# Ranking of the cluster marks one step later, for heads 3 to 15, in a fused clustered-attention and two-layer MLP kernel

## The reference

```python
q_assign = np.argmax(np.einsum('bhsd,hcd->bhsc', q_n, c_n), axis=-1)
k_assign = np.argmax(np.einsum('bhsd,hcd->bhsc', k_n, c_n), axis=-1)
mask = q_assign[:, :, :, None] == k_assign[:, :, None, :]
scores = scale * np.matmul(q, k.transpose(0, 1, 3, 2))
scores = np.where(mask, scores, -1000000000.0)
...
attn = attn / (np.sum(attn, axis=-1, keepdims=True) + 1e-09)
return np.matmul(attn, v)
# then (P(h) / Q(h)) @ w_out with h = x @ w_in, P a cubic and Q = 1 + |b0||h| + |b1|h^2
# then (silu(x @ w_gate) * (x @ w_val)) @ w_out
```

## Time and profile before

| What | Value |
|---|---|
| median of 3 runs | 780.21 us (780.07 to 780.3) |
| the profiled execution, its own time | 779.8 us |
| its span, first to last instruction | 778.0 us |
| busy: PE, DVE, ACT, POOL | 773.2, 569.0, 516.3, 523.1 us |
| DVE busy, attention stretch (slices 1 to 10 of 40) | 90% and more in most slices |
| granted TensorE clock | full in all 40 slices |
| scores of tile 95, the last | at 228.00 us of the span |

### The profile page before, as it was taken

One profiled execution on the slowest core, in us unless ns is written; L12 is line 12 of the kernel. 1 busy time (PEld: TensorE's weight loads), 2 busy tenths in 40 slices (PEclk: granted clock), 3 DMA queues, 4 the chain that ended last, 5 costly groups with the idle time before them and its releaser, 6 DMA issues.

```text
span 778.0 us, 12682 instructions
## 1 busy us (share of the span) xinstructions
PE 773.2 (99%) x4231; PEld 700.5 (90%) x4231; DVE 569.0 (73%) x1046; ACT 516.3 (66%) x960; POOL 523.1 (67%) x457
## 2 busy tenths in 40 slices
PE   9999999999999999999999999999999999999998
PEld 8999999999998888888888888899999999999997
DVE  6999999999998787777777777644544555554554
ACT  7888888888888787686777789553554444333322
POOL 4878999998575997222222488879888975665610
PEclk9999999999999999999999999999999999999999
DMA  8857665463402600000000111341212214211002
GB/s 189 196 138 183 166 175 139 118 163 90 121 14 82 190 0 1 1 0 1 1 0 1 29 44 38 95 122 55 55 28 55 55 29 134 55 42 41 27 1 82
DMA packets 57521, 57.53 MB, mean 74 GB/s; under 512 B 6576, under 2 KB 44272, under 8 KB 57456
## 3 DMA queue, kind: packets, MB, share of 16 engines
q1 hardware_dynamic: 57296, 56.32, 26.9%
q10 hardware_dynamic: 160, 0.39, 0.2%
HBM read 33.59 MB, written 3.15 MB: 47 GB/s over the span
## 4 chain that ended last, share of the span: by engine, by line
PE 98%; DVE 1%; issue 0%; ACT 0%; POOL 0%; POOLq 0%
PE ps L1310 19%; PE ps L1311 19%; PE ps L1312 19%; PE ps L1464 8%; PE ps L1481 4%; PE ps L1408 4%; PE ps L1409 4%; PE ps L1483 4%; PE ps L1407 4%; PE ps L1445 4%; PE ps L1450 4%; PE ps L1515 2%; PE ps L1306 1%; DVE neg_max L1191 1%; DVE probT_lo L1217 0%; PE ps L1419 0%
## 5 line engine op out<-in xcount | busy, mean ns | idle before, releaser
L599 POOL TENSOR_TENSOR den<-den,mag 128x512 f32<-128x512 f32 x48 | 62.4, 1300 | 120.1 <-ACT den L780 119.9
L1312 PE MATMUL ps<-x_hi,w_lo 128*128 128x512 f32 (+1 forms) x384 | 139.5, 363 | 0.0
L658 POOL TENSOR_TENSOR w_lo<-w_raw,w_hi 128x768 fp32r<-128x768 f32 (+1 forms) x48 | 101.6, 2125 | 56.3 <-ACT w_hi L839 56.3
L1310 PE MATMUL ps<-x_hi,w_hi 128*128 128x512 f32 (+1 forms) x384 | 139.4, 363 | 0.0
L1311 PE MATMUL ps<-x_lo,w_hi 128*128 128x512 f32 (+1 forms) x384 | 139.4, 363 | 0.0
L680 POOL TENSOR_SCALAR prob<-prob,row_inv 128x768 f32<-128x768 f32 x96 | 85.9, 912 | 28.0 <-DVE row_inv L1207 27.1
L1217 DVE TENSOR_TENSOR probT_lo<-ps,probT_hi 128x384 fp32r<-128x384 f32 x192 | 97.3, 548 | 6.1 <-ACT probT_hi L927 5.1
L927 ACT ACTIVATE probT_hi<-ps 128x384 fp32r<-128x384 f32 x192 | 83.7, 489 | 22.7 <-PE ps L1464 21.4
L1191 DVE TENSOR_REDUCE neg_max<-ps 128x1 f32<-128x768 f32 x96 | 90.9, 948 | 1.1 <-PE ps L1450 0.8
L907 ACT ACTIVATE prob<-ps,neg_max 128x768 f32<-128x768 f32 x96 | 86.7, 904 | 2.9 <-DVE neg_max L1191 2.7
L1464 PE MATMUL ps<-ident,prob 128*128 128x128 f32 x576 | 79.8, 274 | 0.2
(11 more groups left out here) (150 smaller groups left out, 1988.8 us busy)
## 6 DMA issues: line engine op xcount, KB each, us to landing
w_raw<-in_moe_w_gate SPq DMA_DIRECT2D x48, 128.0 KB, 2.3
w_raw<-in_moe_w_val SPq DMA_DIRECT2D x48, 128.0 KB, 2.6
k_hihi<-qk_hi SPq DMA_DIRECT2D x31, 192.0 KB, 3.3
w_raw<-in_moe_w_in SPq DMA_DIRECT2D x16, 256.0 KB, 3.5
w_raw<-in_moe_w_out SPq DMA_DIRECT2D x16, 256.0 KB, 4.5
qk_raw<-in_q SPq DMA_DIRECT2D x16, 192.0 KB, 4.0
qk_low<-qk_hi SPq DMA_DIRECT2D x16, 192.0 KB, 3.7
qk_low<-qk_lo SPq DMA_DIRECT2D x16, 192.0 KB, 4.1
```

Source lines behind the costliest of these rows:

```text
L658: did(g.tensor_tensor(lo[:, wave, :], raw[:, wave, :], hi[:, wave, :].bitcast(F32), ALU.subtract), s_w2lo)
L1310: mm(dst, hi, m_hi, start=start, stop=False)
L1312: return mm(dst, lo, m_hi, start=False, stop=stop)
```

## The change

In heads 3 to 15 VectorE takes the marks behind the sum of x of step 4, instead of ahead of that step's maximum. Their transposes move from the end of step 4 to the end of step 5, the copy from the start of step 5 to the start of step 0, the rank from step 5 to the end of the transposes of step 0, and the two `cluster` instructions from the end of step 5 to the end of step 0. No instruction is added or removed. SyncE's and GpSimd's orders are the same; SyncE's six DMAs for the rows wait for the later `cluster`.

```diff
-    STAGES = (0, 2, 8, 8, 8, 8, 10, 10, 11, 11)
+    STAGES = (0, 2, 8, 8, 8, 8, 10, 11, 12, 12)
...
                 h = early_at(step, S_CLUSTER)
                 if h is not None:
                     cluster(h)
-                h = steady_at(step, S_MARKS)
-                if h is not None:
-                    marks(h)
                 maximum(step)
...
                 if not products_first(step):
                     x_sum(step)
+                h = steady_at(step, S_MARKS)
+                if h is not None:
+                    marks(h)
                 h = steady_at(step, S_CLUSTER)
                 if h is not None:
                     cluster(h)
...
                 if products_first(step):
                     products(step)
                     turn(step)
-                else:
-                    turn(step)
                     h = steady_at(step, S_RANK)
                     if h is not None:
                         order(h)
+                else:
+                    turn(step)
                     products(step)
```

## The result

The changed kernel takes **781.78 us**, the median of 15 runs (781.49 to 781.96). The kernel before took 780.07 us in 15 runs beside it (779.94 to 780.44). The ratio is 1.0021, with a 95% interval of 1.0014 to 1.0028: the change makes the kernel 1.7 us slower. The forecast was 782.5, with slower as the likeliest outcome.

The account below looks back on a forecast made before the run. TensorE's queue plus its waits was taken as the bound. Terms 1.40 + 0.84 = 2.24, about 2.3, gave 778.0 + 2.3 = 780.3 of span, 782.1 with 1.8 around it, and 0.4 for the median: 782.5 us, range 780.0 to 784.4.

Parts of the forecast that it names:

- Term (c): Cluster instructions behind step 0's low parts: VectorE late through steps 1 to 3, TensorE waits 0.12 in seven heads, 0.84 us.
- term (a): Between step 4's last product and step 5's first: 1.44 us of work left to cover a 1.65 chain, 1.40 us lost.
- The reading of the bound: TensorE's instruction queue plus its waits sets the time; adding and removing no instruction, the change can only move waits.
- The tail's pattern: Steps 88 to 89 and 95, without a rank: transposes to product 0.79 (upper partitions) and 0.72 (lower), waits 0.21 and 0.14.
- The hold of VectorE's sum: Late start of the sum of x, 1.04 against 0.92 behind the low parts, expected to travel with the sum.
- Term (b): Marks' transposes and rank in their new places, steps 5 and 0: same work, marks and copy in time, cost 0.
- Term (d): Six row DMAs on SyncE starting later, still landed before the scores that read them: cost 0.
- Rival 1: Only the lost cover before step 5's product costs; VectorE's slack absorbs the later cluster instructions: 781.6 us, chance 0.23.
- Rival 2: Sum of x, no longer behind the marks, ends in time; seven heads' 0.13 wait goes: 779.3 us, chance 0.10.
- Rivals 3: VectorE as the bound: its 0.4 can't be made up; logits or steps 2 to 4 transposes wait: 785.5 us, chance 0.07.
- 4: The move does nothing, since waits only change place within a head: 780.2 us, chance 0.07.
- the 0.1 in steps 2 to 4: Named test: after even ranks, transposes in steps 2 to 4 should take some 0.1 more than 0.58.

Follow-up runs that it names:

- experiment 8: Changed kernel with VectorE summing x over only 96 of 384 columns, GpSimd filling the rest with repeats (a measurement alone): 778.37 us.
- experiment 5: Changed kernel with one extra 128-column matmul of zeros ahead of the scores in each step 5, 15 in all: 781.91 us.
- experiment 1: Changed kernel with the marks back ahead of the maximum of step 4 on VectorE, all other moves kept: 785.12 us.
- experiment 2: Kernel before with only the rank matmul and the two cluster instructions later; marks, their transposes and the copy in place: 782.42 us.
- experiment 3: Kernel before with only the two cluster instructions a step later, at the end of step 0: 781.51 us.
- experiment 6: Kernel before with the same 15 extra 128-column matmuls of zeros ahead of the scores in each step 5: 780.64 us.

## Why the prediction was right, and where it was not

The forecast of 782.5 was 0.7 above the measured 781.78. Term (c) put in 0.6 that did not come and term (a) 0.07 too little; 0.13 is the kernel before, 780.07 in the longer measurement instead of 780.21, and 0.06 is rounding.

**The reading of the bound** held. No instruction was added, TensorE's work is the same, and all of the 1.7 us is waits that only starts show.

**Term (a), cover lost before the product of step 5**: predicted 1.40, measured 1.47. The tail's pattern was the right stand-in: 0.79 and 0.72 expected, 0.77 to 0.78 and 0.73 to 0.75 found. The 1.44 us of work was right too: in experiment 8, where nothing waits, the distance between the two products is 1.45. Experiments 5 and 8 show that TensorE is idle there and that the chain's length decides, and experiments 1 and 2 that its length does not follow the work beneath it. Head 3, counted with the even ones at 0.08, measured 0.07.

**The hold of VectorE's sum**, with a sum 0.05 sooner in seven heads if it were tied to the marks' place: the hold travelled with the sum, 1.04 against 0.93 behind the low parts. This is as the rule in the Trainium skill, "VectorE: DVE Perf Modes", section "Two Vector instructions with no wait between them", has it, by which such an instruction starts only when all earlier ones have finished.

**Term (b)**: 0 predicted, 0 found. The later marks, copy and rank are waited for nowhere; with even ranks step 0, the rank's new place, is 0.29 us longer from start to start, steps 1 and 4 are 0.09 and 0.13 shorter and step 5 is the same, 0.07 in sum. That is the growth of the wait of term (a), 0.07, and leaves nothing for the moved work.

**Term (c), the cluster instructions behind step 0's low parts**: predicted 7 x 0.12 = 0.84, measured 0.25, all of it in step 86 (0.12 predicted there). This is the step that failed. VectorE's lateness came as worked out. The timeline of the changed kernel has the low parts of step 1 behind an even rank, and the transposes of step 2, in their first two rows:

```profile
139.78 1.02 DVE L1217 TENSOR_TENSOR probT_lo<-ps,probT_hi 128x384 fp32r<-128x384 f32 x2
140.62 0.87 PE L1464 MATMUL ps<-ident,prob 128*128 128x128 f32 x6
...
141.85 1.01 DVE L1217 TENSOR_TENSOR probT_lo<-ps,probT_hi 128x384 fp32r<-128x384 f32 x2
142.73 0.82 PE L1464 MATMUL ps<-ident,prob 128*128 128x128 f32 x6
143.31 0.42 PE L1481 MATMUL ps<-probT_hi,v_split 128*128 128x384 f32 x1
```

The lead of the low parts over the next transposes is 0.84 in the first pair, where it was 1.05 (110.35 and 111.40), and 0.88 in the second, where it was 1.00. So it is 0.21 late at step 1, against 0.22 worked out, but only 0.12 late at step 2, where I had 0.11 of slack, and the transposes behind it still take 0.58 (142.73 to 143.31). I had carried the full lateness to a place that it reaches only in part. By step 4 nearly nothing is left: the low parts at 117.64 lead the transposes at 118.51 by 0.87, against 0.91 before and 0.74 in experiment 3. There the marks still stand ahead of the maximum, and that kernel pays 1.5 us. I take it that the marks' move frees VectorE there, so that (c) is not a term of its own and its price hangs on the other half of the change. This is argued from the starts: no run has the changed kernel with the cluster instructions ahead of the low parts of step 0.

**Term (d), the DMAs**: 0, and no gap at a head's first scores.

**The rivals.** Rival 1 (term (a) alone, 781.6) came nearest in its number, 0.2 under the measured time, but it denied any cost of the cluster instructions, and step 86 has one of 0.25. Rival 2, that the relief works, is half true: by experiment 1 the marks' place is worth 3.3 us once the cover is gone, but that only repairs part of what the moves on TensorE cost. Rivals 3 and 4 fell: no wait appears at the logits, and the two-head stretch is 0.23 longer.

**Tests named beforehand.** The stretch of the earlier trace rows took 14.15 and 14.18 instead of the 14.2 expected; the sum started 0.93 behind the last product in both kinds of head (0.9 expected); the 0.1 in steps 2 to 4 did not come.

## What to carry to other kernels

Small work on the bounding engine that stands between a result and the reuse of its buffer is cover: before moving it, add up what is left between the two by starts and compare that with the chain through the other engines. Where two engines are nearly full, a delay on one is paid only where an order has no slack, so run each part of a change alone: here the cluster instructions alone cost 1.5 us, with the rank's move 2.4, and the whole change 1.7. When the bounding engine reads as 99% busy and small waits are left, take work off the engine that ends them: one small VectorE instruction fewer per half head gave the fastest version that computes the layers, 778.52 us.

## What the runs showed of the hardware

- TensorE reads as busy through waits. With 2.4 us of waits in the starts of step 5, the page says 99% and idle time near zero for these lines; only start-to-start differences, and the filler of experiment 5 that cost 0.1 us instead of 15 x 0.12 = 1.8, show them.
- A VectorE sum in the upper half of the partitions, behind work that begins in the lower, starts 1.04 us behind the low parts instead of 0.93, and the instruction behind it starts 0.60 after it instead of 0.46 (133.32 - 132.72, and 119.03 - 118.57): 0.25 us for where its operands lie.
- The handover from TensorE's last product matmul to ScalarE's copy is 0.37 us from start to start (131.79 to 132.16), from the sum's end to the load of weights 0.12.
- A 128-column matmul of zeros ahead of 384-column ones costs 0.12 us behind a product matmul (experiment 5) and 0.14 behind transposes (experiment 6, 117.39 to 117.53), where six transposes of the same size cost 0.096 each.
